# Attention with a memory, then a mixture of experts: phi of the queries made a pair ahead, and the router's weights times M_prev made behind the first pair's turns

## The chip, the core and the metric

The kernel runs on one core of one Trainium2 chip. The core has five engines with a queue each: TensorE (PE in the profile; PEld is its loading of weights), VectorE (DVE), ScalarE (ACT), GpSimd (POOL) and SyncE (SP), which here only issues DMAs. The engines wait for each other through semaphores. The metric is the device time of one execution in microseconds. Before the change the median of three runs is 517.94 us (513.71 to 518.32).

## What is computed

```python
B, H, S, D = (4, 8, 576, 64)
scores = causal(q k^T / 8);  a = softmax(scores);  local = a @ v
phi(x) = where(x > 0, x, exp(x) - 1) + 1          # = max(x, 0) + min(exp(x), 1)
mem_ret  = phi(q) @ M_prev                        # per head, 64 x 64
mem_norm = phi(q) . z_prev + 1e-6
attn = g * mem_ret / mem_norm + (1 - g) * local   # g = sigmoid(beta), per head
x = attn as [2304, 512]
e_idx = argmax(x @ w_gate)                        # 8 experts, one for each token
out = softmax weight * sigmoid(x @ w_output_gate)[e_idx] * relu(x @ w1[e]) @ w2[e]
```

All of it is float32.

## The kernel before

**Attention, 16 pairs.** A pair `g` is two heads of one batch, 576 queries. There are 16 (`G`), and each engine runs its own loop over `g`. TensorE's order in the turn of the loop for pair `g` is: first scores of `g` (`scores(g, 0)`), `local(g - 2)`, `memory(g - 1)`, the other scores of `g`, the transposes ("turns") of the probabilities that are ready (`EARLY`), `values(g - 1)` (probabilities times v), the scores of the last 64 queries (`tail_scores(g)`), and the turns `(g, 2)` and `(g, 3)` (`LATE`). In every view all of these products show line L1392 and the turns show L1388, so they are told apart by tile: scores write `S` and `O_ps` from `k_pair,q_pair`, `local` writes `TP_ps` from `turn_w,out_T`, `memory` writes `STK` from `m_aug,phi_T`, `values` writes `O_ps` from `probs_T,v_nat`, and the router's product writes `O_ps` from `w_pair,m_turned`.

**Phi.** Three engines make it. ScalarE takes the exponential of the pair's queries (`q_exponential`, L740) between the exponentials of slots 2 and 3. GpSimd makes the positive part (`q_pos`, L573) and bounds the exponential (L575), both in `phi_parts`, and adds the two (`phi`, L587). `phi(g)` waits for the first scores of pair `g + 1` (L584). `memory(g)` stands two steps behind those same scores in TensorE's order. `q_exp` and `q_pos` are single buffers; `phi_T` has two.

**GpSimd's loop.** For each `g` it first adds the memory's and the local part of pair `g - 2` (L618, L622, L632, `x_out`), then in some pairs takes the low part of a weight of the first expert (`low_ahead`, L602, for `g` = 10, 11, 13, 15), for the last pair gathers the tokens of the first two tiles (L605), then runs `phi_parts(g)`, in pairs 9, 12 and 14 `lanes` (L594, L597), and then `phi(g)`. `lanes` waits for VectorE's placing of the tokens.

**SyncE's loop.** For each `g`: in pair 8 the eight pieces of the first expert's weights (L481, 512 KB each), in pairs 14 and 15 pieces of the second expert's, each behind `lo_first` (that is behind `low_ahead`); then `load_v(g)`, the store of `x_out` of `g - 2`, and `load_qk(g + 2)`, which waits for all scores of pair `g` and for `phi(g)`, because it writes into the buffer that both read.

**The router's weights.** `router_weights` multiplies the transposed M_prev of all pairs by the router's two weight matrices, 32 small products into `O_ps`. It stands where `values` would in the first pair, ahead of `tail_scores(0)`. VectorE copies the result into `m_aug` (`memory_weights`, L881, at the end of its first turn), and `memory(0)` waits for that copy.

**After the attention** TensorE runs `local(14)`, the last turn, `values(15)`, transposes the first gathered tile (L1548, which waits for the gather), then `memory(15)` and `local(15)`, and then the experts' tiles with weights split into high and low parts (L1564 to L1566; for the opening half tile L1576 to L1580).

Of the kernel before, what the change touches and what calls it, by code (L numbers as in the profile page):

```python
# [5 lines left out]
def memory_attention_top1_moe(nc, qt, kt, v, m_aug_in, m_t_in, w_pair_in, beta, w1, w2, out):  # L6
# [36 lines left out]
    NS = len(ROWS)  # L43
    SLOTS = [(0, 1, 2), (3, 4), (5, 6), (7,)]
# [33 lines left out]
    def sem(name):  # L78
        return ctx.enter_context(nc.semaphore(name))
# [156 lines left out]
    scored = sem("scored")  # L236
# [71 lines left out]
    def valid(g):  # L308
        return 0 <= g < G
# [114 lines left out]
    with ctx, nc.Block(no_gpsimd_drain=True) as block:  # L424
# [109 lines left out]
        def _(pool):  # L534
# [29 lines left out]
            nc.gpsimd.affine_select(out=below[:, :], in_=below[:, :], compare_op=ALU.is_gt, fill=0.0,  # L564
                                    base=0, pattern=[[1, P]], channel_multiplier=-1).then_inc(r_const, 1)

            def phi_parts(g):
                if not valid(g):
                    return
                pool.wait_ge(ld_first, 32)  # L570
                pool.wait_ge(ld_qk[g % 2], 64 * uses(g))
                wait(pool, phi_done, g)
                nc.gpsimd.tensor_scalar(q_pos[:, :], q_pair[g % 2][:, :], 0.0, None, ALU.max).then_inc(phi_pos, 1)  # L573
                pool.wait_ge(phi_exp, g + 1)
                nc.gpsimd.tensor_scalar(q_exp[:, :], q_exp[:, :], 1.0, None, ALU.min).then_inc(phi_pos, 1)  # L575

            def phi(g):
                if not valid(g):
                    return
                pool.wait_ge(phi_pos, 2 * (g + 1))  # L580
                if valid(g + 1):


                    pool.wait_ge(scored, NS * (g + 1) + len(SLOTS[0]))  # L584

                wait(pool, mem_mm, g - 1)
                nc.gpsimd.tensor_tensor(phi_T[g % 2][:, 0:S], q_exp[:, :], q_pos[:, :], ALU.add).then_inc(phi_done, 1)  # L587
# [16 lines left out]
            def gather(t, s, rows=N):  # L604
# [2 lines left out]
                    in_offset=bass.IndirectOffsetOnAxis(ap=slot_tok_i[:, t:t + 1], axis=0),  # L607
                    bounds_check=rows - 1, oob_is_err=False).then_inc(s, 16)

            for g in range(G + 2):  # L610
                x = g - 2
                if valid(x):
                    u, b, p = x % 2, x // NPAIR, x % NPAIR
                    pool.wait_ge(loc_read, x + 1)
                    at = logits_h[:, b * TPB:(b + 1) * TPB, :, :]
                    new = at if p == 0 else lg_new[:, :, :, :]
                    if x < G - 1:
                        last = nc.gpsimd.tensor_tensor(new, loc_x[:, :, :, D:HC], mem_x[u][:, :, :, D:HC], ALU.add)  # L618
                        if p > 0:
                            last.then_inc(lg_chain, 1)  # L620
                            pool.wait_ge(lg_chain, x - b)
                            last = nc.gpsimd.tensor_tensor(at, at, new, ALU.add)  # L622
                        last.then_inc(lg_added, 1)
                        if p == NPAIR - 1:

                            pool.wait_ge(lg_added, x + 1)
                            nc.gpsimd.tensor_tensor(at[:, :, 0, :], at[:, :, 0, :], at[:, :, 1, :], ALU.add).then_inc(lg_whole, 1)
                    else:

                        pool.wait_ge(hot_done, LAST)  # L630
                    wait(pool, x_stored[u], 16 * 2 * (x // 2))
                    nc.gpsimd.tensor_tensor(x_out[u][:, :, :].rearrange("r t (h c) -> r t h c", h=2), loc_x[:, :, :, 0:D],  # L632
                                            mem_x[u][:, :, :, 0:D], ALU.add).then_inc(x_added, 1)
                    if x < EARLY_TILES:
                        nc.gpsimd.memset(x_ring[:, x, :], 0.0).then_inc(ring_clear, 1)
                if g in LOW_PAIR:
                    low_ahead(LOW_PAIR[g])
                if g == G - 1:

                    for u in range(2):  # L640
                        pool.wait_ge(x_stored[u], 16 * 2 * (LAST * NPAIR // 2))
                    pool.wait_ge(scale_stored[0], 16 * 2 * LAST)
                    pool.wait_ge(ring_clear, EARLY_TILES)
                    pool.wait_ge(early_slots, 1)
                    for t in range(EARLY_TILES):
                        gather(t, gather_first[t], LAST * S)
                phi_parts(g)
                for b in range(LAST):
                    if g == (9, 12, 14)[b]:
                        lanes(b)  # L650
                phi(g)


            pool.wait_ge(lo_done, PC - 1)
# [39 lines left out]
        def _(act):  # L694
# [66 lines left out]
            for g in range(G + 1):  # L761

                for slot in (0, 1, 2):
                    exps(g, slot)
                q_exponential(g)
                exps(g, 3)
                unload(g - 1, NU - 1)
                exps(g, 4)
# [3 lines left out]
                if g == G:  # L772

                    act.wait_ge(turned, len(TURNS))
                    for k in range(KD, PC - 1):
                        high(0, k, 0)
                copy_out(g - 1)
                for b in range(2):
                    if g == (8, 10)[b]:
                        route_exps(b)  # L780
# [541 lines left out]
        def _(pe):  # L1322
# [193 lines left out]
            for g in range(G):  # L1516
# [10 lines left out]
                        turn(g - back, k)  # L1527
                if valid(o):
                    values(o)
                else:  # L1530
                    router_weights()
                tail_scores(g)
                if g == G - 1:
                    early_table()
                for back, k in LATE:
                    turn(g, k)
                if RANK_PAIR.get(g) == 2:

                    pe.wait_ge(masked, NS * (g + 1))
                    rank(2)  # L1540
# [153 lines left out]
```

## Time and profile before

| what | value |
|---|---|
| runs | 517.94 us median (513.71 to 518.32, 3 runs) |
| the profiled execution | 517.84 us, its span 516.1 us |
| PE busy | 475.9 us, 92% of the span |
| PEld, DVE, ACT, POOL busy | 378.9, 303.9, 281.7, 196.3 us |
| attention | about the first 216 us of the span, some 11.5 to 12 us for a pair |
| mean granted clock of TensorE | 0.979 of full |

Read it so: TensorE is busy nearly all the time, and a change to another engine's work counts only where TensorE waits for it, or where such a wait also costs TensorE its clock. The execution that was profiled took 517.84 us, 0.1 us under the median.

### The profile page before, as it was taken

What the parts mean: (1) busy time and instruction counts of PE and PEld (TensorE: products, weight loads), DVE (VectorE), ACT (ScalarE), POOL (GpSimd) and SP (SyncE); (2) the same over time, 40 slices, a digit from 0 to 9 for tenths busy, and PEclk for the clock granted to TensorE, in tenths of its full rate; (3) what the DMA queues carried; (4) which work ended last, traced back from release to release, by engine and by line L of the source; (5) the groups of instructions that cost most, each with busy time, mean ns of one, the idle gap of its engine ahead of it and who ended that gap; (6) DMA issues with size and microseconds to landing.
All of it is one profiled execution on the core that took longest, in us unless ns stands there. A gap on an engine that the chain in (4) does not pass through costs nothing.

```text
span 516.1 us, 11159 instructions
## 1 busy us (share of the span) xinstructions
PE 475.9 (92%) x3920; PEld 378.9 (73%) x3921; DVE 303.9 (59%) x783; ACT 281.7 (55%) x623; POOL 196.3 (38%) x187
## 2 busy tenths in 40 slices
PE   5899999996999898699899999999999999999995
PEld 4666766674677575578688888788888878878884
DVE  4278877886788786569422237972222794893222
ACT  5378877785888775623522226842222883872221
POOL 5336765558677865813422211111111122211100
PEclk9899999998999998889999999999999999999999
DMA  6124433368333363142712106990111496440000
GB/s 207 59 69 119 122 96 97 97 209 307 99 96 99 95 205 104 44 136 85 258 65 80 62 27 217 337 323 24 41 41 41 123 335 256 155 177 35 26 14 21
DMA packets 47359, 64.54 MB, mean 125 GB/s; under 512 B 9678, under 2 KB 28622, under 8 KB 47312
## 3 DMA queue, kind: packets, MB, share of 16 engines
q1 hardware_dynamic: 43232, 54.34, 32.5%
q0 software_dynamic: 4080, 9.60, 5.6%
q8 instruction: 27, 0.44, 0.3%
q14 instruction: 20, 0.16, 0.1%
HBM read 57.03 MB, written 10.90 MB: 132 GB/s over the span
## 4 chain that ended last, share of the span: by engine, by line
PE 60%; POOL 12%; issue 11%; DMA 6%; DVE 5%; SPq 3%; ACT 1%; DVEq 0%; ACTq 0%; POOLq 0%
PE O_ps L1564 7%; PE S L1564 7%; PE O_ps L1566 7%; PE S L1566 7%; PE O_ps L1565 7%; PE S L1565 7%; POOL phi_T L587 4%; PE TP_ps L1591 4%; PE STK L1392 3%; POOL q_exp L575 3%; PE S L1392 3%; POOL q_pos L573 3%; PE O_ps L1392 3%; DVE probs L930 2%; DMA v_nat<-in_v 2%
## 5 line engine op out<-in xcount | busy, mean ns | idle before, releaser
L1255 DVE TENSOR_TENSOR hid_lo<-TP_ps,hid_hi 128x512 fp32r<-128x512 f32 x46 | 31.8, 691 | 112.2 <-ACT hid_hi L841 97.1
L730 ACT ACTIVATE probs<-probs,neg_max 128x128 f32<-128x128 f32 (+2 forms) x144 | 83.0, 581 | 19.4 <-DVE neg_max L930 18.4
L678 POOL DMA_INDIRECT out<-x_ring,slot_tok_i x23 | 25.5, 1107 | 145.1 <-ACT x_ring L849 119.5
L1564 PE MATMUL S<-w_hi,x_hi 128*128 128x512 f32 x180 | 72.3, 402 | 0.0
L1566 PE MATMUL S<-w_hi,x_lo 128*128 128x512 f32 x180 | 70.4, 391 | 0.0
L1565 PE MATMUL S<-w_lo,x_hi 128*128 128x512 f32 x180 | 70.1, 390 | 0.0
L930 DVE CUSTOM_DVE_ANT_0 probs<-S,mask 128x128 f32<-128x128 f32 (+3 forms) x112 | 46.6, 459 | 31.2 <-PE S L1392 31.0
L1564 PE MATMUL O_ps<-w_hi0b,hid_hi 128*128 128x512 f32 x152 | 62.9, 414 | 1.2 <-DVE hid_lo L1255 0.9
L605 POOL DMA_INDIRECT x_ring<-x_tokens,slot_tok_i x28 | 30.7, 1097 | 86.4 <-DMA out<-x_ring,slot_tok_i 69.3
L1566 PE MATMUL O_ps<-w_hi0b,hid_lo 128*128 128x512 f32 x152 | 59.5, 392 | 0.0
L1565 PE MATMUL O_ps<-w_lo0b,hid_hi 128*128 128x512 f32 x152 | 59.3, 390 | 0.0
L1142 DVE TENSOR_TENSOR w_lo<-w_raw,w_hi 128x1024 fp32r<-128x1024 f32 x44 | 51.3, 1218 | 10.5 <-ACT w_hi L759 10.5
L1392 PE MATMUL S<-k_pair,q_pair 64*128 64x128 f32 (+3 forms) x224 | 47.9, 467 | 6.9 <-DMA k_pair<-in_kt 3.9
L1392 PE MATMUL O_ps<-probs_T,v_nat 128*64 128x64 f32 (+4 forms) x576 | 47.2, 319 | 5.8 <-DMA v_nat<-in_v 3.7
L759 ACT ACTIVATE w_hi<-w_raw 128x1024 fp32r<-128x1024 f32 x48 | 48.8, 1053 | 4.5 <-issue 4.5
L849 ACT ACTIVATE x_ring<-O_ps,x_ring 128x512 f32 x21 | 14.4, 684 | 66.4 <-PE O_ps L1566 66.4
L1392 PEld LDWEIGHTS O_ps<-probs_T,v_nat 128*64 128x64 f32 x576 | 32.0, 141 | 20.9 <-issue 15.7
L587 POOL TENSOR_TENSOR phi_T<-q_exp,q_pos 128x576 f32<-128x576 f32 x16 | 23.5, 1468 | 54.1 <-issue 36.2
L1566 PEld LDWEIGHTS S<-w_hi,x_lo 128*128 128x128 f32 x180 | 33.8, 188 | 7.3
L1564 PEld LDWEIGHTS S<-w_hi,x_hi 128*128 128x128 f32 x180 | 33.8, 188 | 6.7 <-issue 0.5
L1565 PEld LDWEIGHTS S<-w_lo,x_hi 128*128 128x128 f32 x180 | 33.9, 188 | 6.3
L1392 PE MATMUL STK<-m_aug,phi_T 64*128 64x81 f32 (+1 forms) x320 | 21.6, 281 | 16.8 <-POOL phi_T L587 16.8
(230 smaller groups left out, 957.7 us busy)
## 6 DMA issues: line engine op xcount, KB each, us to landing
w_raw<-in_moe_w SPq DMA_DIRECT2D x60, 512.0 KB, 5.4
q_pair<-in_qt SPq DMA_DIRECT2D x15, 288.0 KB, 2.9
k_pair<-in_kt SPq DMA_DIRECT2D x15, 288.0 KB, 3.1
v_nat<-in_v SPq DMA_DIRECT2D x16, 256.0 KB, 3.1
x_tokens<-x_out SPq DMA_DIRECT2D x16, 256.0 KB, 2.9
x_ring<-in_moe_w SPq DMA_DIRECT2D x3, 512.0 KB, 8.5
m_aug<-in_m_aug SPq DMA_DIRECT2D x1, 648.0 KB, 6.0
q_tail<-in_qt SPq DMA_DIRECT2D x32, 16.0 KB, 2.9
```

The lines of the kernel that those rows point to most:

```text
L587: nc.gpsimd.tensor_tensor(phi_T[g % 2][:, 0:S], q_exp[:, :], q_pos[:, :], ALU.add).then_inc(phi_done, 1)
L605: nc.gpsimd.indirect_dma_start(out=x_ring[:, t % XR, :], out_offset=None, in_=x_tokens[0:rows, :], in_offset=bass.IndirectOffsetOnAxis(ap= ...
L678: nc.gpsimd.indirect_dma_start(out=out[:, :], out_offset=bass.IndirectOffsetOnAxis(ap=slot_tok_i[:, t:t + 1], axis=0), in_=x_ring[:, t % X ...
L730: last = nc.scalar.activation(pr, pr, ACT.Exp, bias=neg_max[:, slot, h:h + 1], scale=-1.0, accum_out=sums[g % 2][:, at:at + 1])
L759: nc.scalar.activation(w_hi[i][k // KD][:, k % KD, :], raw_piece(e, k), ACT.Copy).then_inc(hi_done, 1)
L930: last = V.tensor_tensor_reduce(row(slot, h * width, (h + 1) * width), rows, hide, -SCALE, 3.0e38, ALU.add, ALU.min, neg_max[:, slot, h:h ...
L1142: V.tensor_tensor(w_lo[i][k // KD][:, k % KD, :], raw_piece(e, k), w_hi[i][k // KD][:, k % KD, :].bitcast(f32), ALU.subtract).then_inc(lo_ ...
L1255: V.tensor_tensor(hid_lo[:, 4 * f:4 * f + 4, :], TPB_ps[:, f, :].rearrange("r (c t) -> r c t", c=4), hid_hi[:, 4 * f:4 * f + 4, :].bitcast ...
L1392: mm = lambda dst, lhs, rhs, start, stop: T.matmul(dst, lhs, rhs, start=start, stop=stop, skip_group_check=True)
L1564: T.matmul(dst, hi, part(i, k)[:, cols], start=first, stop=False)
L1565: T.matmul(dst, hi, part(i, k, True)[:, cols], start=False, stop=False)
L1566: return T.matmul(dst, lo, part(i, k)[:, cols], start=False, stop=last)
```

## The change

Phi of pair `g + 1` is made in GpSimd's turn `g`, and phi of pair 0 ahead of the loop. `phi_parts` is cut into `positive` and `bounded`, with `lanes` between them now. `phi(g)` waits for the first scores of its own pair in place of those of the next. ScalarE takes the exponential of pair `g + 1` behind `copy_out(g - 1)`. `router_weights` runs behind the turns `(0, 2)` and `(0, 3)`. No instruction is added or removed.

```diff
-            def phi_parts(g):
+            def positive(g):
                 if not valid(g):
                     return
                 pool.wait_ge(ld_first, 32)
                 pool.wait_ge(ld_qk[g % 2], 64 * uses(g))
                 wait(pool, phi_done, g)
                 nc.gpsimd.tensor_scalar(q_pos[:, :], q_pair[g % 2][:, :], 0.0, None, ALU.max).then_inc(phi_pos, 1)
+
+            def bounded(g):
+                if not valid(g):
+                    return
                 pool.wait_ge(phi_exp, g + 1)
                 nc.gpsimd.tensor_scalar(q_exp[:, :], q_exp[:, :], 1.0, None, ALU.min).then_inc(phi_pos, 1)
...
                 pool.wait_ge(phi_pos, 2 * (g + 1))
-                if valid(g + 1):
-
-
-                    pool.wait_ge(scored, NS * (g + 1) + len(SLOTS[0]))
+
+
+                pool.wait_ge(scored, NS * g + len(SLOTS[0]))
...
+            positive(0)
+            bounded(0)
+            phi(0)
             for g in range(G + 2):
...
-                phi_parts(g)
+
+                positive(g + 1)
                 for b in range(LAST):
                     if g == (9, 12, 14)[b]:
                         lanes(b)
-                phi(g)
+                bounded(g + 1)
+                phi(g + 1)
...
-                q_exponential(g)
+                if g == 0:
+                    q_exponential(0)
                 exps(g, 3)
...
                 copy_out(g - 1)
+                q_exponential(g + 1)
...
                 if valid(o):
                     values(o)
-                else:
-                    router_weights()
                 tail_scores(g)
...
                 for back, k in LATE:
                     turn(g, k)
+                if g == 0:
+                    router_weights()
```

TensorE's rows in the first pair, before, from the turns `(0, 0)` and `(0, 1)` to the memory's first product:

```order
L1392 MATMUL O_ps<-w_pair,m_turned 64x16 [waits masked,ld_mt]
L1392 MATMUL O_ps<-w_pair,m_turned 64x16 x31
L1392 MATMUL S<-k_pair,q_tail 128x512 [waits turn_dve,masked,consts_dve]
L1392 MATMUL S<-k_pair,q_tail 128x64
L1388 MATMUL TP_ps<-ident,probs 128x64 [waits turn_act,exped]
L1388 MATMUL TP_ps<-ident,probs 128x64 x11
L1388 MATMUL STK<-ident,probs 128x64 [waits exped]
L1388 MATMUL STK<-ident,probs 128x64 x15
L1392 MATMUL S<-k_pair,q_pair 128x128 [waits masked,ld_qk1]
```

And now:

```order
L1402 MATMUL S<-k_pair,q_tail 128x512 [waits turn_dve,masked,consts_dve]
L1402 MATMUL S<-k_pair,q_tail 128x64
L1398 MATMUL TP_ps<-ident,probs 128x64 [waits turn_act,exped]
L1398 MATMUL TP_ps<-ident,probs 128x64 x11
L1398 MATMUL STK<-ident,probs 128x64 [waits exped]
L1398 MATMUL STK<-ident,probs 128x64 x15
L1402 MATMUL O_ps<-w_pair,m_turned 64x16 [waits masked,ld_mt]
L1402 MATMUL O_ps<-w_pair,m_turned 64x16 x31
L1402 MATMUL S<-k_pair,q_pair 128x128 [waits masked,ld_qk1]
```

The router's products have moved behind the 30 other products and turns of the same pair shown here, and stand directly ahead of the first scores of pair 1.

GpSimd's rows in pair 14 and at the head of pair 15, before (the numbers behind the tiles are buffers; `r_lanes` is `lanes(2)`, `w_lo0` is `low_ahead(3)`, the DMAs are the two early gathers):

```order
L597 TENSOR_SCALAR r_lanes<-r_apart 128x640 [waits lanes_apart]
L587 TENSOR_TENSOR phi_T0<-q_exp,q_pos 128x576 [waits mem_mm,scored,phi_pos]
L618 TENSOR_TENSOR lg_new<-loc_x,mem_x1 128x160 [waits loc_read]
L622 TENSOR_TENSOR logits_h<-logits_h,lg_new 128x160 [waits lg_chain]
L632 TENSOR_TENSOR x_out1<-loc_x,mem_x1 128x640 [waits x_stored1]
L602 TENSOR_TENSOR w_lo0<-w_raw3,w_hi0 128x1024 [waits hi_done]
L605 DMA x_ring<-x_tokens,slot_tok_i 128x528 [waits ring_clear,scale_stored0,early_slots,x_stored1,x_stored0]
L605 DMA x_ring<-x_tokens,slot_tok_i 128x528
L573 TENSOR_SCALAR q_pos<-q_pair1 128x576 [waits phi_done,ld_qk1,ld_first]
L575 TENSOR_SCALAR q_exp<-q_exp 128x576 [waits phi_exp]
L587 TENSOR_TENSOR phi_T1<-q_exp,q_pos 128x576 [waits mem_mm,phi_pos]
L618 TENSOR_TENSOR lg_new<-loc_x,mem_x0 128x160 [waits loc_read]
```

And now:

```order
L600 TENSOR_SCALAR r_lanes<-r_apart 128x640 [waits lanes_apart]
L579 TENSOR_SCALAR q_exp<-q_exp 128x576 [waits phi_exp]
L590 TENSOR_TENSOR phi_T1<-q_exp,q_pos 128x576 [waits mem_mm,scored,phi_pos]
L624 TENSOR_TENSOR lg_new<-loc_x,mem_x1 128x160 [waits loc_read]
L628 TENSOR_TENSOR logits_h<-logits_h,lg_new 128x160 [waits lg_chain]
L638 TENSOR_TENSOR x_out1<-loc_x,mem_x1 128x640 [waits x_stored1]
L605 TENSOR_TENSOR w_lo0<-w_raw3,w_hi0 128x1024 [waits hi_done]
L608 DMA x_ring<-x_tokens,slot_tok_i 128x528 [waits ring_clear,scale_stored0,early_slots,x_stored1,x_stored0]
L608 DMA x_ring<-x_tokens,slot_tok_i 128x528
L624 TENSOR_TENSOR lg_new<-loc_x,mem_x0 128x160 [waits loc_read]
```

Behind the gathers nothing of phi is left. Behind `r_lanes` stand now the bounding and the sum of the next pair, where the sum of the same pair stood.

## Rows read from the trace of the kernel before

**Rows 1.** Waits, whole span, then 24 to 208 us: in total, times, longest (us)

```profile
PE STK L1392 <- POOL phi_T L587: 16.8, 16, 3.6
...
PE STK L1392 <- POOL phi_T L587: 11.5, 14, 2.0
```

**Rows 2.** Timeline of a plain pair: start, duration (us), engine, line; idle before in brackets

```profile
68.16 1.19 PE L1392 MATMUL TP_ps<-turn_w,out_T 64*128 64x80 f32 x20
68.89 1.41 POOL L587 TENSOR_TENSOR phi_T<-q_exp,q_pos 128x576 f32<-128x576 f32 x1 [3.92 <-issue]
70.35 1.26 PE L1392 MATMUL STK<-m_aug,phi_T 64*128 64x81 f32 x20 [1.00 <-POOL phi_T L587]
70.78 0.68 ACT L740 ACTIVATE q_exp<-q_pair 128x576 f32<-128x576 f32 x1
72.33 0.56 DVE L930 CUSTOM_DVE_ANT_0 probs<-S,mask 128x384 f32<-128x384 f32 x1 [1.83 <-PE S L1392]
74.13 2.85 PE L1392 MATMUL O_ps<-probs_T,v_nat 128*64 128x448 f32 x36 [0.15 <-DVE neg_max L930]
77.25 0.59 ACT L748 ACTIVATE out_T<-O_ps 128x512 f32<-128x512 f32 x1
78.88 0.87 ACT L717 ACTIVATE probs_T<-TP_ps 128x384 f32<-128x384 f32 x2 [1.03 <-PE TP_ps L1388]
```

**Rows 3.** Timeline of the first two pairs

```profile
12.09 3.60 PE L1392 MATMUL O_ps<-w_pair,m_turned 64*64 64x16 f32 x64 [1.23 <-DMA m_turned<-in_m_t]
20.35 0.41 DVE L881 COPY m_aug<-O_ps 128x256 f32<-128x256 f32 x1
22.09 1.59 PE L1392 MATMUL STK<-m_aug,phi_T 64*128 64x81 f32 x20 [1.65 <-POOL phi_T L587]
27.54 2.85 PE L1392 MATMUL O_ps<-probs_T,v_nat 128*64 128x448 f32 x36 [0.20 <-DVE neg_max L930]
```

**Rows 4.** Timeline, end of pair 7 to pair 9

```profile
102.11 0.76 DVE L930 CUSTOM_DVE_ANT_0 probs<-S,mask_tail 128x576 f32<-128x576 f32 x1
105.57 0.35 SPq L442 DMA_DIRECT2D q_pair<-in_qt  x1
124.76 4.51 PE L1392 MATMUL O_ps<-probs_T,v_nat 128*64 128x448 f32 x36 [3.70 <-DMA v_nat<-in_v]
```

**Rows 5.** Timeline, the waits of pairs 13 and 15 and what stands around them

```profile
170.37 1.26 PE L1392 MATMUL STK<-m_aug,phi_T 64*128 64x81 f32 x20 [1.67 <-POOL phi_T L587]
192.82 1.18 PE L1392 MATMUL TP_ps<-turn_w,out_T 64*128 64x80 f32 x20
194.57 1.40 POOL L587 TENSOR_TENSOR phi_T<-q_exp,q_pos 128x576 f32<-128x576 f32 x1
196.02 1.29 PE L1392 MATMUL STK<-m_aug,phi_T 64*128 64x81 f32 x20 [2.02 <-POOL phi_T L587]
198.51 2.36 POOL L602 TENSOR_TENSOR w_lo<-w_raw,w_hi 128x1024 fp32r<-128x1024 f32 x1
201.26 2.85 PE L1392 MATMUL O_ps<-probs_T,v_nat 128*64 128x448 f32 x36
201.94 0.52 SPq L455 DMA_DIRECT2D v_nat<-in_v  x1
```

**Rows 6.** Page, DMA issues: times, KB each, median us to landing

```profile
v_nat<-in_v SPq DMA_DIRECT2D x16, 256.0 KB, 3.1
```

**Rows 7.** Timeline, end of the attention

```profile
208.58 2.85 PE L1392 MATMUL O_ps<-probs_T,v_nat 128*64 128x448 f32 x36
211.72 0.66 PE L1548 MATMUL S<-ident,x_ring 128*128 128x128 f32 x4 [0.17 <-DMA x_ring<-x_tokens,slot_tok_i]
216.00 2.27 PE L1392 MATMUL STK<-m_aug,phi_T 64*128 64x81 f32 x20 [3.63 <-POOL phi_T L587]
223.76 1.41 PE L1580 MATMUL S<-w_hi,x_lo 128*128 128x512 f32 x4
```

**Rows 8.** Windows (us): PE, PEld, DVE, ACT, POOL busy; granted clock, DMA share, GB/s

```profile
222.00:224.00 2.00, 2.00 (x6) 1.56 (x5) 1.69 (x9) 0.00 (x0) 0.37 (x1) 0.50 0.00 0
```

## The prediction, made before the changed kernel ran

> **What bounds the kernel now.** I read the page's busy times first: TensorE is busy 92% of the span, so only its waits are worth anything. Next the list of waits over the whole span: TensorE's matmuls wait 16 times for GpSimd's phi, 16.8 us together, the longest 3.6 us [rows 1]. That is one wait for each pair. Then the timeline of one plain pair [rows 2]: `local` starts at 68.16 and ends at 69.35, phi starts at 68.89 because it waited for the first scores of this pair, takes 1.41 us, and the memory's product starts at 70.35, 1.00 us after TensorE was free. The bracket before phi ("3.92, issue") says that GpSimd itself had nothing to do for 3.92 us. So phi is late by its own wait, not by GpSimd's load. Then the three places where the wait or its surroundings are longer: the first pairs [rows 3], pair 9, where the values wait for a load and not for phi [rows 4], and pairs 13, 15 and the end [rows 5, 7]. Last the granted clock there: after the wait of 3.63 us TensorE runs at 0.50, that is at 1.2 GHz in place of 2.4 [rows 8].
>
> **What the change does, step by step.** No work is added. Each sum is against the profiled 517.84 us; its span is 516.1 us, so 1.7 us lie around it. The median of the runs is 517.94 us, practically the same.
>
> *Pairs 2 to 14 (the memory's products 1 to 13).* Phi of pair g+1 starts where phi of pair g started, so it is ready a pair (over 10 us) before its reader. TensorE then goes from `local` straight to `memory`. The 14 waits between 24 and 208 us sum to 11.5 us, one of which is the 2.02 us of rows 5; the other 13 give **9.5 us** [rows 1, 5]. Does the next wait give it back? The first masks of the chain behind it had VectorE idle for 1.83 us before them, waiting for TensorE [rows 2], so VectorE follows by 1.0 us earlier and still idles 0.8. ScalarE loses the exponential of the queries (0.68 us) from the stretch ahead of that chain. It gets it back between the copy, which ends at 77.84, and the unloading of the turns at 78.88, which had 1.03 us idle before it: 0.68 fits into 1.03 [rows 2]. That cover is 0.35 us thick; if it goes, each 0.1 us is paid in 14 pairs.
>
> *First pairs.* TensorE ran the router's 3.60 us at 12.09, and everything from there without a break to 20.44 (22.09 less the 1.65 of idle) [rows 3]. In the new order the same block starts some 0.1 us later (VectorE's unloading lets the tail's scores go), in another order, and ends at about 20.5. The router's products end at about 19.7, VectorE's copy of 0.41 us [rows 3] is done by 20.3, just ahead of need, and phi is long there. The memory's product starts at 20.5 and not 22.09: **1.6 us**. Moving the router's products alone gives nothing; it only keeps the copy off the path, by 0.2 us. Behind the 1.65 us wait the path from the memory's product to the values took 27.54 − 22.09 = 5.45 us, in the plain pair 74.13 − 70.35 = 3.78 [rows 2, 3]. Without the wait I expect the shorter one: **1.7 us**; bounds 0 and 1.7.
>
> *Pair 9.* The values wait 3.70 us for v, which is queued behind the first expert's 4 MB, and these behind `load_qk(9)` [rows 4]. That load waited for phi of pair 7 (issued 105.57). Now it waits for the tail's scores of pair 7, which VectorE began to mask at 102.11: the queue moves 3.45 us forward. TensorE itself comes 1.23 us earlier (two waits counted above), so 3.45 − 1.23 = **2.2 us** are new, and 1.4 to 1.5 us of the stall stay. If the transfers were bound by something that does not move, it would be 0; if only TensorE were late, 3.7 − 1.2 = 2.5. The Trainium skill, "DMA: Bandwidth & Descriptors", Queues, rings and completion order, says that descriptors of a queue are consumed in ring order on each DMA engine; by that rule v moves with the pieces ahead of it, the 2.2; if traffic of other queues set it, nothing. The values then took 4.51 us, against 2.85 in every other pair shown [rows 2, 4]. With a stall of 1.4 us I take the clock as kept: **1.7 us**; bounds 0 and 1.7.
>
> *Pair 15.* The wait of 2.02 us goes, and the slow clock behind it: 201.26 − 196.02 = 5.24 against 3.78: **3.5 us** together [rows 2, 5]. But GpSimd now does bounding and sum of the next pair behind `lanes`, where it did only the sum: `lanes` ended at 194.57, then 1.65 + 1.41 (the bounding is as long as in any pair, about 1.65), so all behind it is 1.65 us later. `low_ahead(3)` ends at 202.5 in place of 200.87, and SyncE issues v of pair 15 behind it, at 203.6 in place of 201.94; with 3.1 us to landing [rows 6] that is 206.9. TensorE wants it 3.5 us earlier than the 208.58 of rows 7, at 205.1. A new wait of **−1.8 us**, bounds 0 and −3. Does it cost the clock? The wait of 1.65 us did [rows 3], the one of 1.67 us did not (the pair from 170.37 on ran with matmuls at full length) [rows 5], 2.02 us did. I take it as lost, at the price of rows 4: **−1.6 us**. The Trainium skill, "TensorE: Matmul & The Clock Gate", Part 1, says that the monitor looks at times of its own, not tied to the program; by that rule the same wait costs the clock in one execution and not in another, and the 1.65 and 1.67 us agree. By it each of my clock terms may be there or not, which the bounds hold already.
>
> *End of the attention.* Phi of pair 15 stood behind the two gathers, whose tokens are known late; now it is made ahead of them. The memory's product follows the transposes of the first tile, which end at 212.37: **3.6 us** of wait go [rows 7]. From 216.00 to 225.17 TensorE ran at half clock [rows 7, 8], 9.2 us. At full clock the same matmuls take 4.6, and with the operands that VectorE must make in between I take 4.9: **4.3 us**, bounds 0 and 4.6. The gathers are no obstacle: they start when the early slots are known, which moves with TensorE.
>
> *The experts' part* has no wait for any of this and shifts as a whole.
>
> Sum: 9.5 + 1.6 + 1.7 + 2.2 + 1.7 + 3.5 − 1.8 − 1.6 + 3.6 + 4.3 = 24.7 us. 517.84 − 24.7 = **493.1 us**.
>
> **Rivals.**
> (a) *The clock terms stay away.* TensorE may be granted the half clock at the same places, for a reason that is not the wait. Against it: each slow stretch stands behind a wait of 1.65 us or more. For it: 1.67 us did not slow one. Then 1.7 + 1.7 + 1.5 + 4.3 = 9.2 us go missing: 502.3 us.
> (b) *The pairs' waits come back under another name.* ScalarE's unloading of the turns comes late by the 0.68 us it now has ahead of it, or VectorE becomes the bound in pairs with routing. For it: the cover is only 0.35 us. Against: VectorE and ScalarE both idle in each pair. The 9.5 us are lost: 502.6 us. With (a) as well: 511.8.
> (c) *Slower: a ring between ScalarE and GpSimd.* ScalarE's exponential of pair g+1 waits for phi(g) and for the load of pair g+1, and behind it in ScalarE's queue stand the unloading of the turns, for which TensorE waits. It decides from the point at which either is later than the copy of `out_T`, some 10 us into the pair. If it were, ScalarE would stand in each pair, GpSimd's bounding would wait for ScalarE, and the next phi for that. At 2 us in each of 15 pairs that is 30 − 24.7 = 5.3 us slower: 523.1. Against it: the load is now issued when the pair before ends and lands within about 5 us, and GpSimd idles 3.92 us in a plain pair [rows 2].
> (d) *The change does not do what it says*: phi still comes last before `memory`. That could be only where GpSimd is loaded beyond a pair's time. With `lanes` it is behind by 1.65 us, against the more than 10 us that it is ahead; I exclude it but for (c).
>
> **How the numbers follow.** The forecast has 0.62, (a) 0.16, (b) 0.12, (a) with (b) 0.04, (c) 0.03; 0.03 are left for something else near no change. The forecast's own range is 489 to 498: the new wait for v at 0 and the clock kept there give 489.7, the stall of pair 9 unmoved with its clock lost 497.0. To hold 8 in 10, the range reaches up to (a) and (b): 489 to 503. Runs of this kernel spread by 0.9%, so about 1% is what can be told from no change: faster by over 1% (under 512.7) are the forecast, (a), (b) and both together: 0.94. Within 1%: 0.03. Slower by over 1%: 0.03.
>
> **What would show it.** In the changed profile: no wait of the memory's product for phi in any pair, and plain pairs shorter by 0.6 to 1.0 us. ScalarE's exponential between the copy and the unloading, with a remaining idle of about 0.3 us behind it. The memory's first product near 20.5 us. A wait for v of about 1.4 us in pair 9, and a new one of about 1.8 us before the last pair's values. Full clock from the last transposes to the experts. Wrong would be: a wait of `local` for ScalarE's unloading in each pair; a half clock in the stretch behind the attention in spite of no wait; or the router's copy ending the wait of the first memory's product.

## The result: 499.57 us against 517.79 us

The changed kernel takes 499.57 us (median of 4 runs, 498.20 to 500.94), the kernel before 517.79 us beside it. The ratio of their means is 0.9665, 95% interval 0.9609 to 0.9721. The forecast was 493.1 us. The ratios here and below leave out every execution that is over 1.5% above the fastest of its kernel, such as those of 500.96 us of e7_combo, 497.82 of e8_combo_clear and 493.31 of e11_scalars_first. The profiled executions took 499.52 and 517.84 us: 18.3 us gained, where the sum had 24.7.

One cut shows where the 6.4 us are missing. The memory's product of pair n (here "product n") is in both traces, and stands one pair later in the program than its name (product 14 among the scores of pair 15). The table takes its starts as marks; the last mark is the first `S<-w_hi,x_hi` behind the `w_hi,x_lo` of the first tile.

| Stretch | Before | After | Gained | Forecast |
|---|---|---|---|---|
| start to product 0 | 22.09 | 20.05 | 2.04 | 1.6 |
| product 0 to 1 | 13.48 | 12.83 | 0.65 | 2.25 (wait 0.55, clock 1.7) |
| product 1 to 8 | 81.85 | 74.72 | 7.13 | 4.73 |
| product 8 to 9 | 16.68 | 12.59 | 4.09 | 4.5 (2.2, clock 1.7, wait 0.6) |
| product 9 to 14 | 61.92 | 61.29 | 0.63 | 5.6 (waits 3.6 and 2.0) |
| product 14 to 15 | 19.98 | 20.26 | -0.28 | 1.7 (clock 1.5, then 3.6 - 1.8 - 1.6) |
| product 15 to the experts | 9.00 | 5.10 | 3.90 | 4.3 |
| sum | | | 18.16 | 24.7 |

The rest of the span is 291.1 us before and 290.9 after: the experts shift as a whole. So the plain pairs gave more than forecast, 1.6 us are missing between products 0 and 1, and the main loss is between products 9 and 15.

### The profile page after: what moved, and what is told of

Its sections match the earlier page's. It is cut to its first block, busy times and chain, and to the rows that moved or that the text cites. A ratio compares the mean times of both kernels' runs of the same rounds, so it can differ in the third digit from the quotient of the medians.

```text
span 497.8 us, 11159 instructions
## 1 busy us (share of the span) xinstructions
PE 468.8 (94%) x3920; PEld 378.1 (76%) x3921; DVE 308.1 (62%) x783; ACT 281.7 (57%) x623; POOL 195.2 (39%) x187
## 4 chain that ended last, share of the span: by engine, by line
PE 76%; DVE 13%; issue 6%; DMA 3%; DVEq 1%; ACT 0%; POOL 0%; SPq 0%; ACTq 0%; POOLq 0%
PE S L1402 8%; PE O_ps L1574 8%; PE S L1574 8%; PE O_ps L1576 8%; PE S L1576 8%; PE O_ps L1575 8%; PE S L1575 7%; PE O_ps L1402 7%; DVE probs L940 4%; PE TP_ps L1601 4%; PE STK L1402 4%; PE TP_ps L1402 3%; PE STK L1565 2%; DMA v_nat<-in_v 2%; DVE w_lo L1152 1%
## 5 line engine op out<-in xcount | busy, mean ns | idle before, releaser
L579 POOL TENSOR_SCALAR q_exp<-q_exp 128x576 f32<-128x576 f32 x16 | 26.4, 1652 | 25.1 <-ACT q_exp L748 23.0
L1574 PEld LDWEIGHTS O_ps<-w_hi0b,hid_hi 128*128 128x128 f32 x152 | 28.6, 188 | 6.8 <-issue 1.9
```

What stands on the lines that cost most here:

```text
L1574: T.matmul(dst, hi, part(i, k)[:, cols], start=first, stop=False)
```

## The profile after

The list of waits (in total, times, longest, us) of TensorE, 24 to 200 us, no longer has phi in it [rows 1]. `neg_max` is the row maximum that VectorE takes while it masks a bank of scores; TensorE may overwrite the bank only then. This wait was 2.6 us in total before, 0.7 the longest, and has grown; the wait called "issue", in pair 15, is new; the wait for v, in pair 9, is 2.2 us for 3.7:

```profile
PE S L1402 <- DVE neg_max L940: 6.5, 6, 2.8
PE O_ps L1402 <- issue: 2.9, 1, 2.9
PE O_ps L1402 <- DMA v_nat<-in_v: 2.2, 1, 2.2
```

The timeline of a plain pair, the answer to [rows 2]:

```profile
61.38 0.68 ACT L748 ACTIVATE q_exp<-q_pair 128x576 f32<-128x576 f32 x1
62.52 0.87 ACT L725 ACTIVATE probs_T<-TP_ps 128x384 f32<-128x384 f32 x2 [0.46 <-PE TP_ps L1398]
63.65 1.19 PE L1402 MATMUL TP_ps<-turn_w,out_T 64*128 64x80 f32 x20
63.99 1.41 POOL L590 TENSOR_TENSOR phi_T<-q_exp,q_pos 128x576 f32<-128x576 f32 x1 [0.20 <-POOL q_exp L579]
64.64 1.23 PE L1402 MATMUL STK<-m_aug,phi_T 64*128 64x81 f32 x20
66.55 0.56 DVE L940 CUSTOM_DVE_ANT_0 probs<-S,mask 128x384 f32<-128x384 f32 x1 [0.56 <-PE S L1402]
```

`local` at 63.65 is followed by the memory's product at 64.64, 0.99 us later. Phi at 63.99 is already the next pair's. ScalarE's exponential fits in front of the unloading, with 0.46 us of idle time left (forecast 0.3), and VectorE still idles 0.56 us. The period of the pairs is 10.6 us.

Now pair 10, in the timeline. GpSimd's low part and VectorE's denominators stand side by side:

```profile
126.19 2.35 POOL L605 TENSOR_TENSOR w_lo<-w_raw,w_hi 128x1024 fp32r<-128x1024 f32 x1
126.30 2.27 DVE L948 TENSOR_SCALAR dens<-sums 128x9 f32<-128x9 f32 x1
130.24 0.76 DVE L940 CUSTOM_DVE_ANT_0 probs<-S,mask_tail 128x576 f32<-128x576 f32 x1
131.16 0.93 PE L1402 MATMUL S<-k_pair,q_pair 64*128 64x128 f32 x8 [2.04 <-DVE neg_max L940]
```

The denominators are 9 numbers per partition and take 0.16 us in most pairs. Here they take 2.27 us and end when the low part ends. In the kernel before they came behind the low part (timeline there):

```profile
136.71 2.37 POOL L602 TENSOR_TENSOR w_lo<-w_raw,w_hi 128x1024 fp32r<-128x1024 f32 x1
140.28 0.45 DVE L938 TENSOR_SCALAR dens<-sums 128x9 f32<-128x9 f32 x1
```

In the changed kernel everything behind them in VectorE's queue is late: the mask of the tail at 130.24, hence its maximum, hence TensorE's next scores, which overwrite that bank. Pair 13 is worse (timeline, then the window 167 to 171: busy times of PE, PEld, DVE, ACT, POOL, then the granted clock):

```profile
161.63 2.36 POOL L605 TENSOR_TENSOR w_lo<-w_raw,w_hi 128x1024 fp32r<-128x1024 f32 x1
162.56 1.50 DVE L1016 TENSOR_TENSOR r_diff<-logits_h,r_max 128x40 f32<-128x40 f32 x1
163.96 1.65 POOL L573 TENSOR_SCALAR q_pos<-q_pair 128x576 f32<-128x576 f32 x1
164.09 0.59 DVE L1021 SCALAR_TENSOR_TENSOR r_first<-r_diff,desc 128x40 f32<-128x40 f32 x1
165.57 1.65 POOL L579 TENSOR_SCALAR q_exp<-q_exp 128x576 f32<-128x576 f32 x1
165.60 0.67 DVE L1034 CAST r_so_far<-s_far 128x8 bf16<-128x8 f32 x1
166.99 0.19 PE L1402 MATMUL S<-r_hot,below_bf 128*128 128x40 bf16 x1 [2.80 <-DVE neg_max L940]
```

```profile
167.00:171.00 4.00, 4.00 (x43) 3.82 (x43) 2.57 (x15) 2.44 (x11) 1.63 (x2) 0.57 0.94 319
```

Three ranking instructions that take 0.20, 0.20 and 0.17 us elsewhere take 1.50, 0.59 and 0.67; TensorE waits 2.80 us, where the same place before had 0.71. Behind the wait the clock is 0.57, mostly the lower of its two levels (1.2 GHz, not 2.4): the eight score matmuls and `local` take 1.66 and 2.11 us in place of 0.93 and 1.19, another 1.65 us.

Last, pairs 9 and 15 and the end (timeline; [rows 4, 5, 7]):

```profile
113.33 2.85 PE L1402 MATMUL O_ps<-probs_T,v_nat 128*64 128x448 f32 x36 [2.15 <-DMA v_nat<-in_v]
187.96 2.39 POOL L605 TENSOR_TENSOR w_lo<-w_raw,w_hi 128x1024 fp32r<-128x1024 f32 x1
191.42 0.52 SPq L455 DMA_DIRECT2D v_nat<-in_v  x1
195.45 5.39 PE L1402 MATMUL O_ps<-probs_T,v_nat 128*64 128x448 f32 x36 [2.85 <-issue]
201.74 1.26 PE L1402 MATMUL STK<-m_aug,phi_T 64*128 64x81 f32 x20
206.84 0.39 PE L1574 MATMUL S<-w_hi,x_hi 128*128 128x512 f32 x1
```

The stall of pair 9 is 2.15 us and keeps its clock (the values take 2.85). In pair 15 SyncE issues v behind the piece that waits for the low part; the values wait 2.85 us and then run at half clock, 5.39 us. The last memory product waits for nothing and has full length.

## The experiments

A note on reading the times. The profiled executions differ in their first 30 us. Over the nine kernels with the early phi product 0 starts between 16.86 and 22.65 us (over the four with the late phi between 19.74 and 22.67), and product 0 to 1 takes 11.1 us in five of the nine and 12.7 to 12.9 in four. In those four the router's products and product 0 ran at half clock (timeline of the changed kernel, then of e3_low_first, with the same order there):

```profile
15.08 3.60 PE L1402 MATMUL O_ps<-w_pair,m_turned 64*64 64x16 f32 x64
16.11 2.04 PE L1402 MATMUL O_ps<-w_pair,m_turned 64*64 64x16 f32 x64
```

From product 1 to product 8 all nine of them take 74.7 us. So beside each median stands the time from product 1 to the end of the span, in the one profiled execution: 480.5 us for the kernel before, 464.9 for the changed one. A clock that is kept or lost later in that execution is still in it.

**The change's two halves, apart.** First phi alone, the router's products back at their old place:

```
-                if g == 0:
-                    router_weights()
...
                 if valid(o):
                     values(o)
+                else:
+                    router_weights()
```

> The change with the router's products left where they were, ahead of the first tail scores. My theory: the move of the router's products gives nothing of its own, it only keeps VectorE's copy of their result off the path. Here the copy is at the end of VectorE's first turn as before (done at about 20.8 us), so the memory's first product starts at about 20.8 and not 20.05: 500.2 us against 499.5, a loss of 0.7. Rival: the move is worth more, because the first wait for M_prev's load (1.2 us) and the cold start hang on it: 502 to 503.

497.86 us, ratio 0.9637 (0.9575 to 0.9700); from product 1: 465.9. The same as the whole change. Product 0 starts at 20.01, after the router at 11.85. Then the router's move alone, on the kernel before (the same lines the other way round):

> The kernel before with only the router's products moved. My theory: phi still comes last ahead of the memory's first product, so nothing changes: 517.5 to 518. Rival: about 2 us faster, 516.

515.19 us, ratio 0.9953 (0.9919 to 0.9986); from product 1: 478.6. All waits for phi stand, product 0 starts at 22.67. The gain of some 0.5% is outside the noise, against my expectation, and its cause stays open: in the profiled execution the last product behind its wait of 3.04 us kept its full clock, but that execution took 517.54 us and not the median's 515.19. Phi is the change: with it in place, leaving out the router's move cost nothing (e1_phi_only).

**The low part ahead of the x part.** GpSimd makes `low_ahead` right behind phi rather than behind `x_out`, some 2.5 us earlier:

```
                 x = g - 2
+                if g in LOW_PAIR:
+                    low_ahead(LOW_PAIR[g])
                 if valid(x):
...
-                if g in LOW_PAIR:
-                    low_ahead(LOW_PAIR[g])
                 if g == G - 1:
```

> The change with GpSimd's low part of a weight (2.4 us, pairs 10, 11, 13, 15) ahead of the sum of pair g-2, not behind it. My theory: the new waits of TensorE for VectorE's masks in pairs 10, 11 and 13 (2.04, 1.00, 2.80 us) come from VectorE instructions stretched while GpSimd runs this operation beside them (one of 0.2 us took 2.27). 2.4 us earlier it meets masks that read PSUM, the waits fall to 0.5 us or less each (some 4.9 us), and v of the last pair is issued 2.4 us earlier (its wait of 2.85 us and the clock it costs, 2.5 us, mostly go): 490 us. Rival: VectorE is simply too full in pairs with routing; then only the last pair gains and it is 495.

493.87 us, ratio 0.9553 (0.9508 to 0.9597); from product 1: 461.7. The timeline:

```profile
125.21 0.42 DVE L948 TENSOR_SCALAR dens<-sums 128x9 f32<-128x9 f32 x1
128.22 0.93 PE L1402 MATMUL S<-k_pair,q_pair 64*128 64x128 f32 x8 [0.19 <-DVE neg_max L940]
158.55 1.56 POOL L640 TENSOR_TENSOR x_out<-loc_x,mem_x 128x640 f32<-128x640 f32 x1
158.85 1.31 DVE L1016 TENSOR_TENSOR r_diff<-logits_h,r_max 128x40 f32<-128x40 f32 x1
163.11 0.22 PE L1402 MATMUL S<-r_hot,below_bf 128*128 128x40 bf16 x1 [2.82 <-DVE neg_max L940]
```

In this execution pair 10 waits 0.19 us for 2.04, and the waits of pair 11 and for v of pair 15 are gone too. Pair 13's is not: now `x_out` stands beside `r_diff`, which ends with it. The time is 3.9 us above my 490. Pair 9 waited 2.27 us and lost its clock there, so TensorE came to pair 10 later than it otherwise would; e6_rank_clear below, with the same order there and the clock kept, waits 1.26 us in pair 10.

**The last pairs' values ahead of the weights.** SyncE issues v of pairs 14 and 15 ahead of the second expert's pieces:

```
                 if g >= G - 2:
+                    load_v(g)
                     x = expert_at(1)
...
-                if g > 0:
+                if 0 < g < G - 2:
                     load_v(g)
```

> The change with SyncE loading v of pairs 14 and 15 ahead of the second expert's pieces, and so not behind GpSimd's low part. My theory: the last pair's wait for v (2.85 us) and the half clock behind it (5.39 us in place of 2.85 for the values) go: 494.2 us, and the waits of pairs 10, 11 and 13 stay. Rival: the wait before the last values is not v; then it stays and the time is 499.5.

495.95 us, ratio 0.9590 (0.9547 to 0.9633). The last values start without a wait for v, at 193.00 and at full clock; product 14 to 15 falls from 20.26 to 16.36 us, 3.9 us. The waits of 1.99 and 2.81 us for neg_max stay. From product 1 it is 464.7 us, no less than the changed kernel's 464.9: in this execution the clock stood at 0.50 behind the 1.99 us (130 to 134 us), and product 9 to 14 took 65.01 us for 61.29. The intervals of the two ratios just overlap. So v of pair 15 was late by its place in SyncE's queue, not by its transfer.

**The collision in the kernel before.** If a low part beside the denominators is the cause, it must do harm without the early phi as well:

```
-                if g in LOW_PAIR:
-                    low_ahead(LOW_PAIR[g])
...
                 phi_parts(g)
+                if g in LOW_PAIR:
+                    low_ahead(LOW_PAIR[g])
```

> The kernel before with one thing moved: GpSimd makes the three low parts of pairs 10, 11 and 13 behind the pair's q_pos and q_exp rather than ahead of them. Phi and the router stay as they were before. Theory (a 2.4 us GpSimd instruction that reads and writes SBUF holds up a small VectorE instruction on SBUF that starts beside it): the low parts of pairs 10 and 13 now run at about 140.0 to 142.4 and 176.5 to 178.9, over the denominators that VectorE makes at 140.28 and 176.55; these stretch from 0.16-0.45 us to about 2.1 us, the maxima behind them are late, TensorE waits 1.5 to 2.5 us for them, and since phi in this kernel waits for those same scores, nothing absorbs it: 520.0 to 522.5 us against 517.3. Rival (the late maxima of the changed kernel come from VectorE's own amount of work, GpSimd's neighbour does not matter): denominators stay at 0.16 to 0.45 us, time within 1 us of before.

527.68 us, ratio 1.0237 (1.0195 to 1.0280), over my range, since I had moved one thing too many: the low part of pair 15 went behind the gathers and their waits, SyncE's piece and v behind it, and TensorE stood 12.2 us for the last values. Again, with only the low parts of pairs 10, 11 and 13 moved:

> e5_before_low_late with the low part of pair 15 back at its old place, since in e5 TensorE stood 12.2 us for v of pair 15, whose load was queued behind a weight piece that waits for that part; only the low parts of pairs 10, 11 and 13 stand behind q_pos and q_exp. Theory (stretched denominators make TensorE wait for neg_max, which nothing absorbs): the denominators of pairs 10 and 13 take about 2 us, three waits for neg_max of 1.4 to 2.0 us stand in pairs 10, 11 and 13 as in e5, and the time is 3 to 6 us above before: 519.5 to 523. Rival (all of e5's loss is the 12.2 us in pair 15): within 1.5 us of before.

522.04 us (10 runs), ratio 1.0102 (1.0067 to 1.0138): 5.0 us slower; from product 1: 487.0, 6.5 more than before. Timeline of pairs 11 and 13:

```profile
153.78 1.94 DVE L1026 CAST r_so_far<-s_far 128x8 bf16<-128x8 f32 x1
178.53 2.35 POOL L602 TENSOR_TENSOR w_lo<-w_raw,w_hi 128x1024 fp32r<-128x1024 f32 x1
178.54 2.37 DVE L940 TENSOR_SCALAR dens<-sums 128x9 f32<-128x9 f32 x1
184.04 0.19 PE L1394 MATMUL S<-r_hot,below_bf 128*128 128x40 bf16 x1 [2.69 <-DVE neg_max L932]
```

The three waits are 1.83, 1.72 and 2.69 us, the last above the 2.0 that I had expected; before they were 0.22, 0.34 and 0.71. `dens` of pair 10 takes 2.07 us. No work was added and the early phi is not there: only GpSimd's order has changed, and each held instruction ends with the low part beside it.

**The ranking kept clear in pair 13.** On e3_low_first, GpSimd waits in pair 13 until VectorE has ranked, then makes q_pos, q_exp and phi, and `x_out` behind them:

```
+                    if g == LAST * NPAIR + 1:
+                        pool.wait_ge(hot_done, 2)
+                        positive(g + 1)
+                        bounded(g + 1)
+                        phi(g + 1)
                     wait(pool, x_stored[u], 16 * 2 * (x // 2))
                     nc.gpsimd.tensor_tensor(x_out[u] ...
...
+                if g == LAST * NPAIR + 1:
+                    continue
                 positive(g + 1)
```

> e3_low_first with, in pair 13 alone, GpSimd waiting until VectorE has ranked the batch's tokens (r_so_far written) before its next q_pos, q_exp and phi, and x_out behind these. Theory (of TensorE's wait of 2.82 us for neg_max in pair 13, 2.0 us are three ranking instructions stretched by GpSimd's x_out, q_pos and q_exp: 1.31, 0.59 and 0.67 us where 0.20, 0.20 and 0.17 are usual): they return to 0.2 us each, the wait falls to about 0.8 us; phi comes out later instead, TensorE waits up to 0.7 us for it, and x_out holds up VectorE's loc_x by about 1.7 us. Time 492 to 494.5, so little or no gain over the 493.9 of e3_low_first, but the wait has moved. Rival (the wait is VectorE's own chain in that pair, with the gate's logits late): the wait for neg_max stays at 2.3 us or more.

490.96 us, ratio 0.9489 (0.9427 to 0.9552); from product 1: 457.7, which is 4.1 less than e3_low_first (461.7). Timeline:

```profile
161.12 0.20 DVE L1023 TENSOR_TENSOR r_diff<-logits_h,r_max 128x40 f32<-128x40 f32 x1
162.74 1.65 POOL L573 TENSOR_SCALAR q_pos<-q_pair 128x576 f32<-128x576 f32 x1 [1.89 <-DVE r_so_far L1041]
163.42 0.19 PE L1409 MATMUL S<-r_hot,below_bf 128*128 128x40 bf16 x1 [0.86 <-DVE neg_max L947]
170.23 0.95 PE L1405 MATMUL TP_ps<-ident,probs 64*128 64x64 f32 x14 [2.06 <-DVE loc_x L978]
```

The wait is 0.86 us (forecast 0.8), so of the 2.8 us some 2.0 were stretched instructions. The late `loc_x` costs 2.06 us, as feared; TensorE does not wait for phi. The clock that was lost behind 2.82 us is kept. Of the 4.1 us pair 13 accounts for 1.6 (product 12 to 14: 26.0 us for 27.6); 1.5 are the clock of pair 9, kept here behind a stall of 2.38 us. Pair 10, whose order is e3_low_first's, waits again, 1.26 us, with another instruction held:

```profile
126.70 1.56 POOL L645 TENSOR_TENSOR x_out<-loc_x,mem_x 128x640 f32<-128x640 f32 x1
126.95 1.37 DVE L1028 SCALAR_TENSOR_TENSOR r_first<-r_diff,desc 128x40 f32<-128x40 f32 x1
```

So who is held depends on when TensorE and VectorE arrive, as much as on GpSimd's order.

**Everything together, and given back.** The low parts first, v of 14 and 15 ahead of the second expert, and v of pair 8 ahead of the first:

```
                 if g == NPAIR + 4:
+                    load_v(g)
                     sp.wait_ge(order_done, 1)
...
-                if 0 < g < G - 2:
+                if 0 < g < G - 2 and g != NPAIR + 4:
                     load_v(g)
```

> The changed kernel with the low parts ahead of the x part (e3_low_first), the values of pairs 14 and 15 ahead of the second expert's pieces (e4_v_ahead), and the values of pair 8 ahead of the first expert's pieces, those of pair 9 staying behind them by a shorter way. Theory: pair 15 keeps its clock and has no v wait, pairs 10 and 11 no neg_max wait; in pair 9 the v wait of about 2 us stays if the queue's bytes bound it (same 4 MB ahead of v of pair 9), so 492.0 to 494.5, with at most 1 us better than e3_low_first; if it was the order of v(8) that delayed what is behind, it falls below 1 us and keeps its clock there, 490 to 491.5.

497.56 us, ratio 0.9601 (0.9553 to 0.9649); from product 1: 463.9, which is 2.1 more than e3_low_first alone, where both of my cases had it no slower. (The two ratios' intervals overlap, and the profiled execution was the longest of the four, 500.96 us; e8_combo_clear below, profiled at 490.36 us, has the same pair 10.) The v wait of pair 9 is gone from the list. But TensorE and VectorE now come to pair 10 2 us earlier against GpSimd, which is held there by its own load and `lanes` (timeline, then the window 137 to 140, columns as above):

```profile
127.76 2.36 POOL L605 TENSOR_TENSOR w_lo<-w_raw,w_hi 128x1024 fp32r<-128x1024 f32 x1
128.53 1.62 DVE L948 TENSOR_SCALAR dens<-sums 128x9 f32<-128x9 f32 x1
130.58 1.53 POOL L640 TENSOR_TENSOR x_out<-loc_x,mem_x 128x640 f32<-128x640 f32 x1
130.77 1.40 DVE L1021 SCALAR_TENSOR_TENSOR r_first<-r_diff,desc 128x40 f32<-128x40 f32 x1
134.09 0.93 PE L1402 MATMUL S<-k_pair,q_pair 64*128 64x128 f32 x8 [2.75 <-DVE neg_max L940]
```

```profile
137.00:140.00 3.00, 3.00 (x22) 2.52 (x22) 0.72 (x2) 1.31 (x6) 2.92 (x3) 0.50 0.30 89
```

The 2 us of pair 9 came back as 2.75 us in pair 10, with the half clock behind it. The same with e6's order in pair 13:

> e7_combo with the GpSimd order of e6_rank_clear in pair 13. Theory: as e6_rank_clear against e3_low_first, within 1.5 us of e7_combo either way, the wait for neg_max in pair 13 at about 0.8 us and in its place one for phi below 0.7 us or a late loc_x. Rival (VectorE's own chain): neg_max wait 2.3 us or more, time the same as e7_combo.

494.16 us, ratio 0.9587 (0.9524 to 0.9651), by the ratios not to be told from e7_combo; from product 1: 460.6, or 3.3 us less, 1.9 of them from product 12 to 14, where the clock is kept. The waits are 2.76 in pair 10, 0.87 and 2.06 in pair 13.

**The collisions taken away.** First the low parts of pairs 10 and 11 one pair later:

```
-    LOW_PAIR = {10: 0, 11: 1, 13: 2, 15: 3}
+    LOW_PAIR = {11: 0, 12: 1, 13: 2, 15: 3}
```

> e7_combo with the low parts of pairs 10 and 11 one pair later (pairs 11 and 12), still ahead of the x part. Theory (e7_combo lost what it saved in pair 9 because TensorE and VectorE came to pair 10 2 us earlier against GpSimd, so that the low part met the denominators again, 1.62 us, and x_out met r_first, 1.40 us): the denominators of pair 10 are back at 0.16 us, x_out still meets the ranking, so the wait for neg_max falls from 2.75 to 1.0-1.5 us; pair 13 keeps 2.8. 491 to 495, 1 to 3 us below e7_combo (497.6). Rival (that wait is VectorE's own chain): 2.3 us or more stay.

492.62 us, ratio 0.9505 (0.9438 to 0.9571); from product 1: 459.4. Pair 10 waits 1.07 us for 2.75, pair 13 3.09. I was wrong in who is held: the denominators still took 1.31 us, now beside `x_out`, and `r_first` was free. Then, in pairs 10 and 13, q_pos and q_exp ahead of `x_out`:

```
+                    if g in (10, 13):
+                        positive(g + 1)
+                        bounded(g + 1)
                     wait(pool, x_stored[u], 16 * 2 * (x // 2))
                     nc.gpsimd.tensor_tensor(x_out[u] ...
...
-                positive(g + 1)
+                if g not in (10, 13):
+                    positive(g + 1)
...
-                bounded(g + 1)
+                if g not in (10, 13):
+                    bounded(g + 1)
```

> e10_low_shift with, in pairs 10 and 13, q_pos and q_exp (GpSimd tensor_scalar, one SBUF input) ahead of x_out (tensor_tensor, two SBUF inputs), so that they and not x_out or the low part stand beside VectorE's ranking. Theory (two-input GpSimd instructions hold a small VectorE instruction until they end, one-input ones only for 0.2 to 0.5 us): r_diff of pair 13 and r_first of pair 10 fall from 1.3-1.5 us to at most 0.6 us, the waits for neg_max in pairs 10 and 13 fall to at most 0.5 and 1.5 us, phi stays in time: 487 to 491. Rival (any GpSimd instruction holds VectorE alike, so only who stands there changes): r_diff or r_first at 1.3 us or more beside the 1.65 us q_pos, waits as in e10_low_shift, time the same as that.

484.02 us (483.78 to 493.31), ratio 0.9402 (0.9321 to 0.9484), below my range; from product 1: 454.1, 10.8 us less than the change as it was made. It has the lowest median here, though its interval overlaps those of e6_rank_clear and e10_low_shift. Part of it is the clock, which never fell in the profiled execution (mean 0.999); in the executions of 489.82 and 493.31 us it was 0.985 and 0.991. Timeline of pair 13:

```profile
155.22 1.65 POOL L573 TENSOR_SCALAR q_pos<-q_pair 128x576 f32<-128x576 f32 x1
155.51 0.42 DVE L1021 TENSOR_TENSOR r_diff<-logits_h,r_max 128x40 f32<-128x40 f32 x1
155.97 0.20 DVE L1026 SCALAR_TENSOR_TENSOR r_first<-r_diff,desc 128x40 f32<-128x40 f32 x1
158.25 0.19 PE L1407 MATMUL S<-r_hot,below_bf 128*128 128x40 bf16 x1 [1.57 <-DVE neg_max L945]
```

`r_diff` takes 0.42 us beside q_pos and not the 1.3 to 1.5 that it takes beside `x_out` or the low part, and `r_first` 0.20. The wait is 1.57 us, a little over the forecast, and keeps the clock. Pair 10 waits less than 0.3 us.

## Why the prediction held, and where its sum did not

The mechanism was right: phi is out of TensorE's way everywhere, and e1_phi_only shows that it is the whole gain. The time lies in the stated 489 to 503 us because that range was widened to hold the rivals; the forecast's own, 489 to 498, ends 1.6 us below it. By its steps:

- **Pairs 1 to 8: mis-sized, too small.** 7.13 us where the waits add to 4.73. The step from `local` to the memory's product was 1.81 us before (56.68 to 58.49) and is 0.99 now, 0.82 less for a wait of 0.62. So a wait costs 0.2 us more than its length: `local` lasts 1.19 us, and without a wait the next group starts before that time is over. Seven pairs at 0.2 us make 1.4 us, and between products 1 and 8 the waits for neg_max fell from 1.46 to 0.51 us. With the 4.73 that is 7.08 of the 7.13 us.
- **First product: right in kind** (2.04 for 1.6). The wait of 1.65 us is gone; that the number fits is partly luck, since the start of product 0 varies by 3 us among the kernels with the late phi. In e1_phi_only, without the router's move, it starts at 20.01, so the 0.2 us that the move should save do not show. **The clock behind it: wrong in this execution**: 12.83 us from product 0 to 1, where five of the nine kernels above have 11.1. I had put the half clock down to the wait for phi; here no wait stands there, and product 0 took 2.27 us (in e3_low_first 1.35), behind the router's products that were already at half clock. Both lengths occur with the same start of the program (e3_low_first 11.12, e6_rank_clear 12.85), so this term had to be a chance and not a sum.
- **Pair 9: nearly right**: 4.09 for 4.5; the stall is 2.15 and not 1.4 to 1.5 us, the clock is kept.
- **Products 9 to 14: the step that failed.** I took these pairs as plain ones and wrote that VectorE follows by 1 us and still idles 0.8 [rows 2]. In pairs with routing it does not. The waits for neg_max grew by 4.9 us (to 6.3, of which 5.84 in pairs 10, 11 and 13, from 1.5 in that stretch before), and the clock in pair 13 took 1.65. Rival (b) had the right name, "VectorE becomes the bound in pairs with routing", but gave it no mechanism. The mechanism is the instruction that runs on GpSimd at the same time: behind the turns with `lanes` (9 and 12), with bounding and phi of the next pair ahead of it, and in pair 9 with the load of the next pair's queries late, GpSimd reaches the low part later against TensorE. In pair 10 it is at 6.0 us behind product 9 (126.19 to 120.19) where it was 2.6 (136.71 to 134.10), in pair 13 at 6.4 us behind product 12 where it was 2.9, and `dens` and the ranking meet it. In the kernel before the same pair of instructions missed each other: the low part ended at 139.1, `dens` came at 140.28. In the runs with the order changed (e3, e6, e9, e11) what is stretched is each time what then stands beside a GpSimd instruction.
- **Pair 15: right in kind, too small.** The wait for v is 2.85 and not 1.8 us, the clock behind it costs 5.39 - 2.85 = 2.54 and not 1.6. e4_v_ahead gives 3.9 of these back.
- **End: right**: 3.90 for 4.3; the wait and the half clock of [rows 8] are gone.

The Trainium skill, "SBUF — State Buffer", SBUF: two separate sides, has the rule that I had left out of the sum: VectorE and GpSimd share a port pair, and a VectorE instruction with two SBUF inputs or in its faster two-port mode that starts second beside a GpSimd instruction which reads SBUF is locked out until that one has ended. The traces agree for the low part and `x_out` (2.27 us beside 2.35, 2.37 beside 2.35, 1.31 beside 1.56). For q_pos and q_exp, which read SBUF too, they agree that VectorE is held, but not for the whole instruction: `r_first`, with two SBUF inputs, took 0.59 us when it started 0.13 us into q_pos (the changed kernel, pair 13) and 0.20 when it started 0.75 us into it (e11_scalars_first).

The Trainium skill, "TensorE: Matmul & The Clock Gate", Part 1, says that the clock's monitor keeps times of its own, not tied to the program. The runs agree: a stall of 2.27 us in pair 9 lost the clock (e3_low_first, values 4.47 us), one of 2.38 us at the same place kept it (e6_rank_clear, 2.85 us).

## What to carry to other kernels

When work moves off the critical path to an engine that is mostly idle, ask beside whom it will now stand. An instruction of 9 numbers can cost as much as the 1024-column one on the neighbouring engine, and it shows as a wait for a third. So look, before the change, at the minimum and maximum of the small VectorE instructions in the list of groups, and lay GpSimd's two-input instructions beside stretches in which VectorE reads PSUM (its masks kept their 0.69 us there). And a gain at one place can move two engines into step at the next: e7_combo removed a 2 us stall and got 2.75 us back.

## What the hardware showed that was not expected

- What started beside GpSimd's two-input instructions (`x_out`, the low part, phi) and goes from SBUF to SBUF (`dens`, `r_diff`, `r_first`, `r_so_far`) was held until 0.03 to 0.06 us behind their end, in every profile here (`dens` of pair 10, 2.27 us for 0.16). Two kinds were not held in the same stretches: reciprocals (0.22 us at 161.75 in the changed kernel, inside the low part) and reductions (`r_max`, 0.20 us at 162.33).
- Beside q_pos and q_exp (one input, 1.65 us) there are two holding stretches and a gap. `r_first`, `r_diff`, `r_hot`, `dens` and `r_so_far`, when they started in the first 0.5 us, ended 0.68 to 0.73 us behind the start of q_pos or q_exp. Those that started at 0.7 to 1.0 us took their usual 0.16 to 0.20 us. From 1.02 us on `dens`, `r_so_far` and `s_over` were held until its end (`r_so_far` 0.65 us at 140.28 in the changed kernel), while `r_first`, `r_hot` and `r_out`, with two inputs, were not (0.19 to 0.20 us). No run here shows why.
- VectorE's masks (0.69 us) and `mem_x` (0.99 us), which read PSUM, took the same beside a low part (e3_low_first, 154.8 to 156.9 us) as anywhere.
- The same order of work took 11.1 or 12.7 to 12.9 us from product 0 to 1 in different executions, and 74.7 us from product 1 to 8 in all of them: a mark behind the start tells more than a median of three.
